# Turning the spatial weights on VectorE and moving a token block by DMA in a fused attention, gating and mixing kernel

## The reference

```python
# 1 attention, 8 heads of 64; keys kept: pos_k < n_global (8), or 0 <= pos_q - pos_k < n_local (96)
scores = q @ k.T / sqrt(64) - slopes[h] * dist          # everything else -1e9
x = softmax(scores) @ v                                 # heads side by side: B x 768 x 512
# 2 gating unit
h = relu(x @ w_in); u, v = h[..., :512], h[..., 512:]
v_n = (v - mean(v)) / sqrt(var(v) + 1e-6)
x = (u * (einsum('ts,bsd->btd', w_spatial, v_n) + b_spatial[None, :, None])) @ w_out
# 3 mixer
u = x + ((x.T @ U @ V).T)                               # over tokens, rank 32
out = u + relu(u @ w_ch1) @ w_ch2                       # 512 -> 2048 -> 512
```

## Time and profile before

| | before |
|---|---|
| median of 3 runs | 559.49 us (557.4 to 560.1) |
| the profiled execution | 562.82 us, span 560.7 us |
| TensorE busy | 533.7 us (95%) |
| VectorE busy | 289.5 us (52%) |
| ScalarE busy | 174.3 us (31%) |
| GpSimd busy | 112.0 us (20%) |
| mean granted TensorE clock | 0.98 of 2.4 GHz |
| chain that ended last | 80% TensorE, 10% VectorE, 4% GpSimd, 3% issue |

### The profile page before, as it was taken

One profiled execution on the slowest core, in us unless ns is written; L12 is line 12 of the kernel. 1 busy time (PEld: TensorE's weight loads), 2 busy tenths in 40 slices (PEclk: granted clock), 3 DMA queues, 4 the chain that ended last, 5 costly groups with the idle time before them and its releaser, 6 DMA issues.

```text
span 560.7 us, 7652 instructions
## 1 busy us (share of the span) xinstructions
PE 533.7 (95%) x2728; PEld 418.3 (75%) x2728; DVE 289.5 (52%) x845; ACT 174.3 (31%) x429; POOL 112.0 (20%) x134
## 2 busy tenths in 40 slices
PE   7688999899999999999989999999999999999996
PEld 5455666567777788878768888888888888888884
DVE  5748888857775534689822265523146524011012
ACT  4755665645555533332311101021010102101010
POOL 5884000000000001498389500000000000000000
PEclk8969999989999999999989999999999999999999
DMA  7975454545514000055223100002000002000002
GB/s 179 226 158 130 102 102 105 119 97 130 122 47 129 29 30 0 2 168 161 84 76 112 39 0 1 0 1 75 1 0 2 0 2 75 1 0 1 0 1 79
DMA packets 45835, 36.25 MB, mean 65 GB/s; under 512 B 29504, under 2 KB 39744, under 8 KB 45792
## 3 DMA queue, kind: packets, MB, share of 16 engines
q1 hardware_dynamic: 39776, 19.34, 15.6%
q0 software_dynamic: 3216, 11.63, 6.9%
q10 hardware_dynamic: 2800, 4.72, 2.9%
HBM read 32.54 MB, written 3.15 MB: 64 GB/s over the span
## 4 chain that ended last, share of the span: by engine, by line
PE 80%; DVE 10%; POOL 4%; issue 3%; DMA 2%; ACT 1%; DVEq 0%; POOLq 0%; ACTq 0%
PE ps L1255 66%; PE ps L1228 5%; PE ps L1299 4%; PE ps L1272 4%; DVE uT_first L1051 2%; DMA w_raw<-in_moe_w_in 2%; POOL win_lo L464 2%; DVE pr L923 1%; PE ps L1390 1%; POOL win_hi L462 1%; DVE uT_lo L1058 1%; DVE wspT_lo L1010 1%; DVE sc L907 1%; DVE gv_lo L991 1%; POOL small L486 0%
## 5 line engine op out<-in xcount | busy, mean ns | idle before, releaser
L1176 DVE SCALAR_TENSOR_TENSOR hT_lo<-ps,hT_hi 128x512 fp32r<-128x512 f32 x48 | 33.2, 692 | 171.4 <-ACT hT_hi L773 171.4
L773 ACT ACTIVATE hT_hi<-ps 128x512 fp32r<-128x512 f32 x48 | 28.8, 599 | 228.2 <-PE ps L1255 228.2
L597 ACT ACTIVATE pr<-sc,small 128x256 f32<-128x256 f32 (+1 forms) x96 | 46.2, 483 | 52.2 <-DVE small L907 46.8
L907 DVE CUSTOM_DVE_ANT_0 sc<-ps,bias 128x256 f32<-128x256 f32 (+1 forms) x96 | 35.0, 400 | 22.8 <-PE ps L1272 21.2
L1255 PE MATMUL ps<-win_hi,xT_hi 128*128 128x512 f32 x96 | 40.9, 427 | 0.0
L1051 DVE STREAM_TRANSPOSE ys<-tokens 32x128 f32<-32x128 f32 x128 | 38.7, 302 | 1.8
L1255 PE MATMUL ps<-uT_hi,w1a_hi 128*128 128x512 f32 x96 | 38.0, 396 | 1.0 <-DVE uT_lo L1058 1.0
L1255 PE MATMUL ps<-win_hi,xT_lo 128*128 128x512 f32 x96 | 38.5, 401 | 0.0
L1255 PE MATMUL ps<-win_lo,xT_hi 128*128 128x512 f32 x96 | 38.4, 400 | 0.0
L1255 PE MATMUL ps<-uT_lo,w1a_hi 128*128 128x512 f32 x96 | 38.1, 397 | 0.0
L1255 PE MATMUL ps<-uT_hi,w1a_lo 128*128 128x512 f32 x96 | 38.0, 396 | 0.0
(11 more groups left out here) (154 smaller groups left out, 1096.4 us busy)
## 6 DMA issues: line engine op xcount, KB each, us to landing
w_raw<-in_moe_w_ch POOLq DMA_DIRECT2D x16, 512.0 KB, 4.0
wsp<-in_moe_w_spatial ACTq DMA_DIRECT2D x12, 384.0 KB, 3.7
vn<-in_v SPq DMA_DIRECT2D x12, 256.0 KB, 3.7
out<-ys SPq DMA_DIRECT2D x12, 256.0 KB, 2.2
qk_late<-in_q SPq DMA_DIRECT2D x24, 112.0 KB, 3.5
qk_late<-in_k SPq DMA_DIRECT2D x24, 112.0 KB, 3.7
vp<-in_v SPq DMA_DIRECT2D x10, 224.0 KB, 4.5
w_raw<-in_moe_w_in POOLq DMA_DIRECT2D x4, 512.0 KB, 6.0
```

Source lines behind the costliest of these rows:

```text
L597: act.activation(pr[:, k % 3, e, 0:w], sc[:, k % 2, e, 0:w], ACT.Exp, bias=nmax[:, k % 2, e:e + 1], scale=-1.0, accum_out=sums[:, k % 3, e ...
L773: act.activation(hT[0][:, n % 2, :], h1_ps(n), ACT.Relu).then_inc(s["hT_hi"], 1)
L907: dve.tensor_tensor_reduce(out=sc[:, k % 2, e, 0:w], in0=scores_ps(k, e)[:, 0:w], in1=bias[:, 2 * p + e, WINDOW - w:WINDOW], scale=-SCALE, ...
L1176: dve.scalar_tensor_tensor(hT[1][:, n % 2, :], h1_ps(n), 0.0, hT[0][:, n % 2, :], ALU.max, ALU.subtract).then_inc(s["hT_lo"], 1)
```

## The change

- **Spatial weights, second batch.** TensorE's 36 `wsp_transpose` blocks for batch 1 are gone. The weights are loaded as 32x32 blocks in turned block order (`load_blocks`: four DMAs of 128-byte runs for each t), VectorE transposes within the blocks (`turn_wsp`, two of 128x384 for each t), and `wsp_hi` and `wsp_lo` read the result from SBUF. Even t lives in `wsp` and `wspT`, odd t in `wsp_late` and `wspT_late`; in `products(1)` the work is for t + 2.
- **First token block.** For tokens 0 to 3 of batch 0 the 16 small transposes are replaced by one of 128x512 (`turn_rows`, into the single buffer `u_rows`) and 16 DMAs by SyncE that put the 32x32 blocks in place. `turn_rows(n)` stands behind `layer_norm(1, n + 2)`; it waits until the 16 moves of n - 1 have landed. `uT_hi` and `uT_lo` come one turn of the loop earlier than before.
- **Two banks.** `x_ps` alternates for tiles up to PAIRED - 1 = 7.
- **Entry order.** `u_v_late` runs for tiles 4 and 5 of batch 1 v(4), v(5), u(4), u(5); ScalarE's `relus` follows it.
- **Start of the mixer.** `hidden(0)` stands ahead of `low_rank(1, 4)`.

```diff
@@ -51,6 +51,7 @@
+PAIRED = (ALONE + NP) // NP
@@ -214,8 +219,21 @@
+        hT_at = place[0]
...
+        hT_end = place[0]
...
+        ys_end = place[0]
+        place[0] = hT_at
+        wspT_late = hi_lo("wspT_late", [P, NT, P])
+        u_rows = sb("u_rows", [P, CM, TURNS, TURN])
+        assert place[0] <= hT_end
+        place[0] = hT_at + NT * P * 4
+        wsp_turned.append(sb("wsp_turned_late", [P, NT, P]))
+        place[0] = hT_end
+        wsp_late = sb("wsp_late", [P, S])
+        assert place[0] <= ys_end
+        place[0] = ys_end
@@ -251,7 +269,7 @@
         def x_ps(tile):
-            return ps[:, 6 + (tile % 2 if tile < NT else 0), :]
+            return ps[:, 6 + (tile % 2 if tile < PAIRED else 0), :]
@@ -265,6 +283,14 @@
         def wsp_ps(h, wide):
...
+        def wsp_blocks(t):
+            return (wsp_late if t % 2 else wsp)[:, :].rearrange("p (a k c) -> p a k c", a=TURNS, c=TURN)
+        def wspT_of(b, t):
+            return wspT_late if b and t % 2 else wspT
@@ -343,6 +369,7 @@
+        blocks_d = w_sp.rearrange("(i r a) (k y c) -> i y r (a k) c", a=TURNS, r=TURN, y=TURNS, c=TURN)
@@ -422,6 +449,12 @@
+            for n in range(TB):
+                sp.wait_ge(s["u_blocks"], n + 1)
+                for x in range(TURNS):
+                    for y in range(TURNS):
+                        sp.dma_start(uT_first[y * TURN:(y + 1) * TURN, :, n * P + x * TURN:n * P + (x + 1) * TURN],
+                                     u_rows[x * TURN:(x + 1) * TURN, :, y, :]).then_inc(s["u_moved"], 16)
@@ -581,6 +614,12 @@
+            def load_blocks(t):
+                if t < NT:
+                    for y in range(TURNS):
+                        act.dma_start(wsp_blocks(t)[y * TURN:(y + 1) * TURN, :, :, :].rearrange("p a k c -> p (a k) c"),
+                                      blocks_d[t, y, :, :, :]).then_inc(s[f"blocks_loaded{t % 2}"], 16)
@@ -652,12 +691,22 @@
                 if t:
...
-                u_relu(b, t, wide)
+                if t == NT - 1:
+                    gv_hi(b, t)
+                    u_relu(b, t - 1, wide)
+                if t != NT - 2:
+                    u_relu(b, t, wide)
             def wsp_hi(b, t, h, wide):
-                wait(act, "wsp_transposed", b * (2 * NT) + 2 * t + h + 1)
-                act.activation(wspT[0][:, h * HALF:(h + 1) * HALF, :].rearrange("p k n -> p (k n)"),
-                               wsp_ps(h, wide), ACT.Copy).then_inc(s["wspT_hi"], 1)
+                half = slice(h * HALF, (h + 1) * HALF)
+                if b:
+                    act.wait_ge(s["wsp_turned"], 2 * t + h + 1)
+                    src = wsp_turned[t % 2][:, half, :].rearrange("p k n -> p (k n)")
+                else:
+                    wait(act, "wsp_transposed", 2 * t + h + 1)
+                    src = wsp_ps(h, wide)
+                act.activation(wspT_of(b, t)[0][:, half, :].rearrange("p k n -> p (k n)"), src,
+                               ACT.Copy).then_inc(s["wspT_hi"], 1)
@@ -679,21 +728,28 @@
                 if j == 0:
...
-                act.wait_ge(s["u_turned"], tb * TB + j + 1)
+                if tb == 0:
+                    act.wait_ge(s["u_moved"], 16 * TURNS * TURNS * (j + 1))
+                else:
+                    act.wait_ge(s["u_turned"], (tb - 1) * TB + j + 1)
...
                 for t in range(NT):
                     for h in range(2):
-                        if t + 1 < NT:
+                        if b and t + 2 < NT:
+                            wsp_hi(b, t + 2, h, True)
+                        if b == 0 and t + 1 < NT:
...
-                    if t + 2 < NT:
+                    if b:
+                        load_blocks(t + 4)
+                    elif t + 2 < NT:
...
-                    if b and 0 < t <= TB:
-                        uT_hi(0, t - 1)
+                    if b and t < TB:
+                        uT_hi(0, t)
@@ -753,19 +818,28 @@
-                    wsp_hi(after, (t + 1) % NT, 0, False)
+                    if t + 1 < NT:
+                        wsp_hi(0, t + 1, 0, False)
...
-                    wsp_hi(after, (t + 1) % NT, 1, False)
-                    load_wsp((t + 2) % NT)
+                    if t + 1 < NT:
+                        wsp_hi(0, t + 1, 1, False)
+                    if t + 2 < NT:
+                        load_wsp(t + 2)
+                    elif t + 2 == NT:
+                        load_blocks(0)
...
+                load_blocks(1)
...
                 for t in range(1, NT):
...
-                gv_hi(1, NT - 1)
+                    if t <= 2:
+                        for h in range(2):
+                            wsp_hi(1, t - 1, h, True)
+                        load_blocks(t + 1)
@@ -1004,10 +1078,24 @@
+            def turn_wsp(t):
+                dve.wait_ge(s[f"blocks_loaded{t % 2}"], 16 * TURNS * (t // 2 + 1))
+                if t % 2 == 0:
+                    dve.wait_ge(s["mixed"], NT + max(t - 1, 0))
+                elif t > 1:
+                    dve.wait_ge(s["mixed"], NT + t - 1)
+                for h in range(2):
+                    half = slice(h * HALF, (h + 1) * HALF)
+                    dve.transpose(wsp_turned[t % 2][:, half, :].rearrange("p k (r a) -> p a k r", a=TURNS),
+                                  wsp_blocks(t)[:, :, half, :]).then_inc(s["wsp_turned"], 1)
             def wsp_lo(b, t, h, wide):
...
-                hi, lo = [w[:, h * HALF:(h + 1) * HALF, :].rearrange("p k n -> p (k n)") for w in wspT]
-                dve.tensor_tensor(lo, wsp_ps(h, wide), hi, ALU.subtract).then_inc(s["wspT_lo"], 1)
+                half = slice(h * HALF, (h + 1) * HALF)
+                hi, lo = [w[:, half, :].rearrange("p k n -> p (k n)") for w in wspT_of(b, t)]
+                src = wsp_turned[t % 2][:, half, :].rearrange("p k n -> p (k n)") if b else wsp_ps(h, wide)
+                dve.tensor_tensor(lo, src, hi, ALU.subtract).then_inc(s["wspT_lo"], 1)
@@ -1039,6 +1127,13 @@
+            def turn_rows(n):
+                wait(dve, "u_ready", n + 1)
+                dve.wait_ge(s["u_moved"], 16 * TURNS * TURNS * n)
+                dve.transpose(u_rows[:, :, :, :].rearrange("p c y r -> p (c y) r"),
+                              tokens[:, n, :].rearrange("p (m r) -> p m r", r=TURN)).then_inc(s["u_blocks"], 1)
@@ -1061,20 +1156,19 @@
                 for t in range(NT):
...
-                    for h in range(2):
-                        if t + 1 < NT:
+                    if b and t + 2 < NT:
+                        turn_wsp(t + 2)
+                    if b == 0 and t + 1 < NT:
+                        for h in range(2):
...
-                    for x in range(2):
-                        if b and t < TB:
-                            turn_tokens(t, x)
+                    if b and 0 < t <= TB:
+                        uT_lo(0, t - 1)
...
-                    for x in range(2, TURNS):
-                        if b and t < TB:
-                            turn_tokens(t, x)
-                    if b and t >= 2:
-                        uT_lo(0, t - 2)
+                    for h in range(2):
+                        if b and t + 2 < NT:
+                            wsp_lo(b, t + 2, h, True)
@@ -1155,20 +1254,29 @@
-                    wsp_lo(after, (t + 1) % NT, 0, False)
+                    if t + 1 < NT:
+                        wsp_lo(0, t + 1, 0, False)
...
-                    wsp_lo(after, (t + 1) % NT, 1, False)
+                    if t + 1 < NT:
+                        wsp_lo(0, t + 1, 1, False)
...
                 for t in range(1, NT):
+                    if t <= 2:
+                        turn_wsp(t - 1)
...
+                    if 2 <= t:
+                        turn_rows(t - 2)
+                    if 2 <= t <= 3:
+                        for h in range(2):
+                            wsp_lo(1, t - 2, h, True)
@@ -1291,7 +1399,7 @@
                 if p == 0:
...
-                    wait(pe, "xT_lo", tile if tile > NT else tile - 1)
+                    wait(pe, "xT_lo", tile if tile > PAIRED else tile - 1)
@@ -1354,6 +1462,16 @@
+            def u_v_late(b, t, wide):
+                for q in (0, 1):
+                    u_v_piece(b, t, q, wide)
+                for q in (2, 3):
+                    if t == NT - 1:
+                        u_v_piece(b, t - 1, q, wide)
+                for q in (2, 3):
+                    if t != NT - 2:
+                        u_v_piece(b, t, q, wide)
@@ -1465,16 +1584,20 @@
                 for t in range(NT):
-                    a, after = ALONE + 3 * t, (t + 1) // NT
+                    a = ALONE + 3 * t
...
+                    if t == 1:
+                        wait(pe, "xT_lo", PAIRED)
                     if t:
...
-                    wsp_transpose(after, (t + 1) % NT, 0, False)
+                    if t + 1 < NT:
+                        wsp_transpose(0, t + 1, 0, False)
...
-                    wsp_transpose(after, (t + 1) % NT, 1, False)
+                    if t + 1 < NT:
```

(22 more changed lines are left out.)

34 lines of the change are left out of this document (21 added, 13 removed).

## The result

| | before | after |
|---|---|---|
| median of 4 runs each | 559.24 us (557.4 to 560.1) | 577.79 us (575.06 to 580.11) |
| ratio, with 95% interval | | 1.033 (1.030 to 1.036) |
| span of the profiled execution | 560.7 us | 578.2 us |
| mean granted clock | 0.980 | 0.970 |

The changed kernel is 18.5 us slower. The forecast was 7.0 us slower, and its range ended at 573.5. Its direction was right, its size was not.

What follows compares the result with a forecast made beforehand. The prediction took TensorE, busy for 95% of the span, as the bound. It summed -3.2 - 3.3 - 4.7 + 16.5 + 1.7 + 0 = +7.0 us onto 559.5: 566.5 us, range 558.5 to 573.5.

Steps and rivals of the forecast that it cites:

- Part 5: First token block by DMA: chained moves delay gv_lo(1, 5) before the second mixing's last products, 16.5 us lost.
- link: One step of the first token block's chain: row transpose, 16 issues, landing; 10.4 us, bounds 8.7 and 11.7.
- the 16.5: Loss in us before the second mixing's last products: gv_lo(1, 5) ending at 255.95 in place of 239.45.
- Rival (a): First token block's moves hidden behind the layer norms, link under about 5.5 us: 548.3 to 549.2 us, chance 0.09.
- 1.7 for the clock: Loss in us from low granted clock after TensorE's idle time in the second mixing, 0 to 2.5.
- -2.6 for the transposes: Gain in products(1) from four groups of weight transposes taken off TensorE, 0.65 us each.
- Part 1: Two banks for turned tokens in probs_v: idle time and low clock before the first mixing go, 3.2 us gained.
- Rival (d): The bank pair gains nothing because VectorE paces that stretch: +3.2 us, within the forecast's range; no separate chance.
- Parts 2 and 6: 36 weight transposes off TensorE, 3.3 us gained; the spatial weights' turning on VectorE counted as 0.
- Part 6: Spatial weights turned on VectorE: its products(1) turn, 7.5 us with waits, fits in 7.8; 0, bounds -0.8 and +3.
- Rival (c): Chain plus wsp_lo and uT_lo waiting for GpSimd in products(1), +11 us at most: 572 to 578 us, chance 0.10.
- Part 3: End of the second products, hidden(0) first and uT_lo one turn earlier: 4.7 us gained, 2.8 if clock falls elsewhere.

Runs made afterwards that it cites:

- e1: The changed kernel with four buffers for the transposed rows in place of one, so no transpose waits for earlier moves: 552.40 us, ratio 0.986.
- e9: The changed kernel, single buffer kept, with four moves per block over 128 partitions in place of sixteen, blocks landing permuted: 554.23 us, ratio 0.989.
- e11: The changed kernel with each of the 64 moves reading 512 B rows of w_spatial from HBM, destination as in e6: 569.3 us, one run.
- e3: The changed kernel with each move reading 512 contiguous bytes per partition, destination still strided: 576.08 us, ratio 1.029.
- e6: The changed kernel with each move's 512 bytes per partition contiguous at source and destination, blocks landing permuted: 576.60 us, ratio 1.030.
- e4: The kernel before with only the second bank for turned tokens added: 558.26 us, ratio 0.997.
- e7: e1 with the second batch's spatial weights turned by TensorE again, as in the kernel before: 552.07 us, ratio 0.985.
- e8: e1 with block loads queued behind gT_hi and uT_hi, and the four uT_lo moved to the loop's last two turns: 550.09 us, ratio 0.983.
- e2: The changed kernel without moves, the first token block turned by 64 small VectorE transposes inside the second products again: 566.37 us, ratio 1.013.

## Why the forecast's direction was right and its size wrong

**The chain (Part 5): right in kind, wrong by one price.** The forecast had a link of 10.4 us: transpose 1.1 + 0.1 + 15 x 0.46 + landing 2.3. Measured, from one transpose to the next: 13.6, 12.3 and 12.4 us, of which 0.71 + 15 x 0.645 + 1.85 = 12.2. The issue is the step that failed. The forecast took 0.46 us for each of 15 issues, and the runs show 0.645. I took 0.46 from a DMA that reads HBM and kept 0.46 as the dear end of that term, although no row showed one that reads SBUF. It cost 0.185 x 15 = 2.8 us a link. The shorter transpose and landing gave 0.85 back. The first link held one issue of 1.74 us on top. Three links together: 38.3 us in place of 31.2, so +7.1. `gv_lo` took 2.54 in place of 1.4, +1.1. A shorter last transpose takes 0.4 off again. Added to the 16.5 that is 24.3; the stage lost 24.2. Shown by e1 (no chain, no loss), e9 (a quarter of the issues, nearly no loss) and e11 (HBM's price, the forecast's link). e3 and e6 exclude the layout.

Rival (a) had the condition right, a link under some 5.5 us. e9's starts are 5.9, 5.6 and 4.5 us apart, and its time is 554.2. The Trainium skill (DMA: Bandwidth & Descriptors, Issuing engines are not separate DMA queues) says that issuing is usually small relative to the DMA itself. Here 16 issues took 10.3 us and the landing 1.85, so the measurement decides against it for many small moves.

**Low clock and first turn of the loop: +3.8 us.** The forecast had 1.7 for the clock and -2.6 for the transposes, -0.9 in all. The stage came out at +2.9. It lies in the loop's beginning: from the mixing's last token tile to the second `gated` transposes it takes 14.4 us, in e1 10.3; from there on 32.8, in e1 33.5. The clock stayed at 0.50 from 246 through 266 us, and the 7.3 us that TensorE was busy in them ran at half pace. In that same stretch ScalarE's queue holds four block loads ahead of `gT_hi(1, 0)`:

```profile
263.49 4.76 ACTq L620 DMA_DIRECT2D wsp<-in_moe_w_spatial  x4
268.30 0.60 ACT L713 ACTIVATE gT_hi<-ps 128x512 fp32r<-128x512 f32 x1 [4.29 <-issue]
```

One of the four takes 2.49 us; in e1 all four take 2.70. `gT_hi` and `gT_lo` are late by that, the two `wspT_lo` behind them meet a GpSimd subtraction, and TensorE waits 0.6 us for `gT_lo` and 1.2 for the second gate. e3's trace has the same chain and the same 0.50 up to 265.5 us, but there the four loads take 3.16 us and the two `wspT_lo` 1.02:

```profile
263.03 3.16 ACTq L620 DMA_DIRECT2D wsp<-in_moe_w_spatial  x4
...
267.48 1.02 DVE L1098 TENSOR_TENSOR wspT_lo<-wsp_turned,wspT_hi 128x384 fp32r<-128x384 f32 x2
```

TensorE then waits for neither, and the 14.4 us are 11.7. So of the 4.1 us that the changed kernel has above e1 here, e3 has 1.4 as well, and 2.7 come only where the loads are late. By start times those 2.7 are 2.2 for the two waits and 0.4 for two more products at the low clock. e1 itself waits 0.8 us for `gT_lo` here, so clock and queue don't simply add up. These are single executions, and the changed kernel's is the slowest of its four.

**The banks (Part 1): -2.5 in place of -3.2.** The idle time and the low clock of the earlier trace rows went, as said. The new stall was put at 0.45 us, on `biased`; it is 1.0 us, on ScalarE's copy of `pT`. The clock stayed at 1.00 after it. Rival (d), no gain from the banks, doesn't hold in the traces (2.5 us in both the changed kernel and e4).

**The transposes taken from TensorE (Parts 2 and 6): right by count, wrong by cover.** A group's price of 0.65 us holds: e7's turn is 8.4 us and e8's 7.75. But in e1 the gain doesn't arrive, and `gated`, `x_lo` and `gT_lo` are waited for instead. Part 6 summed VectorE's turn to 7.5 us, inside 7.8, and took that for cover. What counted was the order within the turn: `uT_lo` and ScalarE's 2.7 us of block loads stand ahead of the steps TensorE waits for. With both behind, the same sum fits (e8; which of the two counted for more is open). I had also costed ScalarE's block loads at 1.8 us a group and at nothing on the path; they were 2.7, and in `window` they delay `pT`, `x_hi` and the gate, which took 0.5 of the 0.66 us expected there. e8 shows it: with `load_blocks(0)` behind these steps, 7.3 us later, the 0.5 us wait for the gate is gone, and the stage is 80.34 us long, 0.7 under the kernel before.

Had the moves been hidden, the forecast said 548.3 to 549.2. e1 measured 552.4. Of the 3.6 us between, the banks have 0.7, the window 0.6, and the stage with the loop 2.1 (43.8 us in place of the 41.7 forecast).

**"19 us of small transposes worth little" (Part 5): wrong in this kernel.** In the kernel before they lay beside TensorE's work: its loop is 42.5 us long, and e7's, which has none of them, 42.0. But the question was what they cost beside the turned weights, and e2 gives 14.0 us. The two parts of the change support each other; I priced each against the kernel before.

**Contention with GpSimd.** `gv_lo` started 0.34 us after a GpSimd subtraction and ended 0.54 us after its end; the two `wspT_lo` took 3.62 us across another one, and 1.02 from 287.48 on, with GpSimd idle. This agrees with the Trainium skill (SBUF — State Buffer, Who interferes with whom): a VectorE instruction with two SBUF inputs is held off while GpSimd has the ports. Rival (c) named this and got the time right, 572 to 578, by the wrong sum. It wanted up to 11 us in the loop, and the stage lost 3.8 for all causes. Its time came from the chain. In e8 such pairs still take 1.9 to 3.9 us while GpSimd splits, and TensorE waits 0.2 us in the loop: what contention costs depends on what is queued behind it.

**The end (Part 3): -4.65 in place of -4.7**, all as said: `hidden(0)` starts at 307.03, 0.35 us behind the transposes, and nothing is late.

## What to carry to other kernels

Where many small DMAs stand in a chain, count issues first: their number times the issuing engine's price, not the bytes, and give a price for a kind that no row shows a dear end well above the nearest row. A buffer that is refilled only when all its moves have landed turns that sum into a wait; four buffers or a quarter of the moves each removed it here. When work goes to an engine that has room, look at what it is queued in front of, and price parts that share an engine together.

## What the runs showed of the hardware

- An issue on SyncE took 0.60 us with a source in SBUF and 0.42 us with one in HBM, to the same place in SBUF. Neither run length (128 or 512 B, 0.60 and 0.59), nor bytes (16 or 64 KB), nor partitions (32 or 128) changed the 0.60.
- ScalarE's issue of a block load with 24 runs of 128 B per partition took 0.67 us. Four of them took 2.7 us in e1 and 4.76 us in the changed kernel, both beside SyncE's moves, and one issue alone took 2.49 us there. In e9 four took 2.66 us after the last move, and in e2, which has no moves, 3.49. So SyncE's moves are not needed for a slow one; what makes it is open.
- VectorE turned 128x512 in 0.71 us and two of 128x384 in 1.6, where `q_turned` took 1.1 us for 128x512.
- One idle stretch of 1.0 us left the granted clock at 1.00, where the one of 2.0 us before had been followed by 0.57. After those of 10.4 and 11.5 us it was 0.50 until about 266 us.
